# Order of the first heads of a fused attention and two-MLP kernel: six edits to its hand-written start

## The reference

```python
scores = q @ k.T / 8; scores = where(causal, -1e9, scores); scores -= scores.max(-1)
a = exp(scores); a /= a.sum(-1) + 1e-9
local = a @ v
phi = where(q > 0, q, exp(q) - 1) + 1
mem_out = (phi @ M_prev) / (phi @ z_prev + 1e-6)
x = g * mem_out + (1 - g) * local              # g = sigmoid(beta), per head
h = relu(x @ w_in); x = (s * h * h + b) @ w_out            # 2304 x 512, width 2048
h = x @ v_in; solu = h * softmax(h)                        # width 1024
out = layernorm(solu) * g_ln @ v_out
```

## Time and profile before

| | |
|---|---|
| median of three executions | 870.0 us |
| the profiled execution's own time | 870.0 us |
| its span, first to last instruction | 868.3 us |
| busy: TensorE, VectorE, ScalarE, GpSimd | 99%, 57%, 37%, 30% |
| granted TensorE clock, mean | 1.000 |
| TensorE waiting for VectorE's maxima (L948), whole span | 2.9 us in 7 waits |

### The profile page before, as it was taken

One profiled execution on the slowest core, in us unless ns is written; L12 is line 12 of the kernel. 1 busy time (PEld: TensorE's weight loads), 2 busy tenths in 40 slices (PEclk: granted clock), 3 DMA queues, 4 the chain that ended last, 5 costly groups with the idle time before them and its releaser, 6 DMA issues.

```text
span 868.3 us, 13401 instructions
## 1 busy us (share of the span) xinstructions
PE 855.3 (99%) x4966; PEld 755.7 (87%) x4966; DVE 492.5 (57%) x1036; ACT 317.6 (37%) x572; POOL 257.3 (30%) x371
## 2 busy tenths in 40 slices
PE   8999999999999999999999999999999999999998
PEld 7899999999888888888888889999998888888886
DVE  7766666666548865433443344344757655656664
ACT  6656566565432223222322222232243323232322
POOL 5656656565569992000000000000600000000000
PEclk9999999999999999999999999999999999999999
DMA  8665757564403322000000000000210000000000
GB/s 148 149 139 124 162 126 157 131 151 97 118 25 103 112 89 62 1 1 0 1 1 1 0 1 1 1 1 1 89 57 13 12 25 25 24 24 24 13 24 36
DMA packets 86359, 49.27 MB, mean 57 GB/s; under 512 B 65056, under 2 KB 73248, under 8 KB 86304
## 3 DMA queue, kind: packets, MB, share of 16 engines
q1 hardware_dynamic: 83760, 47.94, 22.8%
q10 hardware_dynamic: 2544, 0.59, 0.4%
HBM read 27.28 MB, written 4.72 MB: 37 GB/s over the span
## 4 chain that ended last, share of the span: by engine, by line
PE 89%; DVE 7%; issue 2%; ACT 1%; POOL 0%; POOLq 0%; ACTq 0%
PE ps_h L1265 8%; PE ps_h L1267 8%; PE ps_h L1266 8%; PE ps_y L1280 7%; PE ps_y L1282 7%; PE ps_y L1281 7%; PE ps_v L631 7%; PE ps_hid L1541 4%; PE ps_r L1570 4%; PE ps_s L546 4%; PE ps_hid L1543 4%; PE ps_hid L1542 4%; PE ps_r L1572 4%; PE ps_r L1571 4%; DVE spent L948 3%
## 5 line engine op out<-in xcount | busy, mean ns | idle before, releaser
L1384 DVE TENSOR_TENSOR xT<-xT 128x512 f32<-128x512 f32 (+1 forms) x80 | 60.3, 754 | 133.7 <-ACT xT L1340 133.7
L1265 PE MATMUL ps_h<-x_hi,win 128*128 128x512 f32 (+1 forms) x320 | 117.7, 368 | 0.0
L1267 PE MATMUL ps_h<-x_hi,win 128*128 128x512 f32 (+1 forms) x320 | 117.5, 367 | 0.0
L1282 PE MATMUL ps_y<-g_hi,wout 128*128 128x512 f32 (+1 forms) x320 | 117.5, 367 | 0.0
L1281 PE MATMUL ps_y<-g_lo,wout 128*128 128x512 f32 (+1 forms) x320 | 117.5, 367 | 0.0
L1266 PE MATMUL ps_h<-x_lo,win 128*128 128x512 f32 (+1 forms) x320 | 117.5, 367 | 0.0
L1280 PE MATMUL ps_y<-g_hi,wout 128*128 128x512 f32 (+1 forms) x320 | 117.4, 367 | 0.0
L631 PE MATMUL ps_v<-v_raw,pT 128*128 128x65 f32 (+1 forms) x960 | 107.6, 254 | 1.2 <-DVE t_loc L1046 1.2
L631 PEld LDWEIGHTS ps_v<-v_raw,pT 128*128 128x128 f32 (+1 forms) x960 | 101.3, 173 | 6.9 <-issue 4.7
L948 DVE CUSTOM_DVE_ANT_0 spent<-ps_s,mask 128x576 f32<-128x576 f32 (+4 forms) x160 | 81.6, 539 | 42.4 <-PE ps_s L546 41.6
L767 ACT ACTIVATE pT<-ps_x 128x512 f32<-128x512 f32 (+3 forms) x128 | 64.1, 501 | 94.5 <-PE ps_x L613 93.6
(11 more groups left out here) (164 smaller groups left out, 1685.7 us busy)
## 6 DMA issues: line engine op xcount, KB each, us to landing
stacked<-cut SPq DMA_DIRECT2D x56, 288.0 KB, 5.2
out<-res SPq DMA_DIRECT2D x18, 256.0 KB, 2.0
v_raw<-in_v SPq DMA_DIRECT2D x32, 128.0 KB, 3.2
stage<-in_moe_w_in SPq DMA_DIRECT2D x16, 256.0 KB, 2.7
stage<-in_moe_w_out SPq DMA_DIRECT2D x16, 256.0 KB, 2.6
k_raw<-in_k SPq DMA_DIRECT2D x28, 128.0 KB, 2.5
q_raw<-in_q SPq DMA_DIRECT2D x28, 128.0 KB, 3.6
stage<-in_moe_w_in SPq DMA_DIRECT2D x4, 512.0 KB, 3.8
```

The lines of the kernel that those rows point to most:

```text
L1265: pe.matmul(out, hi, x_hi[:, k, 0:n], start=(k == 0), stop=False)
L1267: ins = pe.matmul(out, lo, x_hi[:, k, 0:n], start=False, stop=(k == KT - 1))
L1282: ins = pe.matmul(out, wout[:, f, LO, w], g_hi[:, r, 0:n], start=False, stop=(f == FT - 1))
L1384: dve.tensor_tensor(r, r, r, ALU.mult).then_inc(square_done, 1)
```

## The change

Six edits, all in the written-out start.

1. GpSimd: `mask_weights(0, 1)` goes ahead of `spread_maxima(1)`, which now waits for 4 masked tiles, and `cut_queries(2)` ahead of `mask_weights(0, 3)`.
2. TensorE: `keep_warm` does twice as many matmuls where its output has fewer than 128 partitions, that is in its third call.
3. TensorE: `cross(0, 3)` goes ahead of `first_rows(2)`.
4. TensorE: `cross(3, 2)` goes behind `turn_queries(4)` and `third_rows(5)`.
5. VectorE: both `low_keys` of pair 1 go behind `first_rows(2)`.
6. VectorE: `second_rows(5)` goes ahead of `cut_keys(4)`.

```diff
--- before.py
+++ after.py
@@ -429,11 +429,11 @@
 
         mask_weights(0, 0)
         round_queries(2)
-        pool.wait_ge(q_hi_done, 1)
+        mask_weights(0, 1)
+        pool.wait_ge(tri_done, 4)
         spread_maxima(1)
-        mask_weights(0, 1)
+        cut_queries(2)
         mask_weights(0, 3)
-        cut_queries(2)
         features(0)
 
         mask_weights(1, 0)
@@ -481,7 +481,7 @@
                 pe.matmul(ps_s[:, 0:P], ident[:, :], ident[:, :], start=True, stop=True)
 
         def keep_warm(into):
-            for _ in range(WARM_BETWEEN):
+            for _ in range(WARM_BETWEEN * (2 if into.shape[0] < P else 1)):
                 pe.matmul(into, ident[:, 0:into.shape[0]], ident[:, :], start=True, stop=True)
 
         def turn_keys(p):
@@ -696,8 +696,8 @@
         turn_queries(2)
         third_rows(1)
         cross(0, 2)
+        cross(0, 3)
         first_rows(2)
-        cross(0, 3)
         turn_keys(2)
 
         cross(1, 0)
@@ -737,9 +737,9 @@
         second_rows(5)
         cross(3, 1)
         weigh_values(2, (2,))
-        cross(3, 2)
         turn_queries(4)
         third_rows(5)
+        cross(3, 2)
         weigh_values(2, (3,))
         cross(3, 3)
         memory(2)
@@ -1078,11 +1078,11 @@
         first_rows(1)
         low_queries(1, 1)
         second_rows(1)
+        third_rows(1)
+        first_rows(2)
+
         low_keys(1, 0)
-        third_rows(1)
         low_keys(1, 1)
-        first_rows(2)
-
         second_rows(2)
         cut_keys(2)
         third_rows(2)
@@ -1100,8 +1100,8 @@
         scale_local(0)
 
         first_rows(5)
+        second_rows(5)
         cut_keys(4)
-        second_rows(5)
         third_rows(5)
         scale_memory(2)
```

## The result

Six executions of the changed kernel took 874.13 to 878.68 us, median 875.35; six of the kernel before 869.97 to 870.48, median 870.25. The ratio is 1.0062, 95% interval 1.0046 to 1.0079. The forecast was 872.8, range 871.2 to 874.0: the direction held, the time lies outside. The spread is news too: 4.5 us, for 0.5 before. The profiled execution, a seventh, took 878.92 us, its span is 877.2. The fastest, 874.13 us, was the only one of the seven at full clock; its span is 871.2, so 2.9 us lie outside it, where the kernel before had 1.7.

A forecast was written before the change was run, and what follows sets the result against it. TensorE was taken to bound the loops, with only the first 48 us a chain of hand-overs. 1.49 us at the start plus 1.30 at pair 4 gave 2.79 on 870.0: forecast 872.8 us, range 871.2 to 874.0.

The forecast's parts named there:

- The replay of the hand-overs: First 48 us: same durations in the new order, hand-over latencies from neighbouring rows; lateness moves everything behind, sum 2.79 us.
- The doubled dummies: Third keep_warm, ahead of cross(0,0): five more matmuls make it 1.13 us later, bounds 0.76 and 1.13.
- the unnamed 0.37 us before 17.89: Gap on TensorE ahead of cross(0,0), not the old dummies' time; at most this could swallow new dummies.
- The low_keys: VectorE behind first_rows(2): 1.52 us for the pair, next maximum at 26.15 for 24.66, 1.49 us late; 0.34 without dummies.
- GpSimd's order: Last mask of head 0 late, weigh_values(0) stalls 0.83 us; costed at nothing, since TensorE has slack there.
- its cover is VectorE's lateness: The mask stall costs nothing because second_rows(3) waits for VectorE anyway; without that, up to 0.8 us.
- The second place: Pair 4, 44 to 48 us: cut_keys(4) late, turn_queries(4) at 47.18 for 46.23; costs 1.30 us, bounds 1.1 and 1.5.
- the first place: The start through heads 0 to 2, up to second_rows(3): all engines 1.49 us late, dummies included.
- the third rival: "The clock falls": new TensorE pauses bring half pace, 4 us of work lose 2; 874.8 us or more, chance 0.08.
- a pause of 0.96 us: Longest earlier TensorE pause counted, at 21.49, followed by full pace; set against new pauses of 0.5 to 1.4 us.
- Only one of the two places pays: Dummies hidden at the start, or VectorE far enough ahead at 44 us: 871.6 us, chance 0.14.
- not slower: Maxima first shortens VectorE's chain, shown by the 24.66 maximum starting before 24.7: 869.6 to 870.4 us, chance 0.08.

The follow-up runs named there:

- e13: The changed kernel run once more, beside three other kernels on one chip: median 876.73 us, ratio 1.0073, clock falls in 4 of 6.
- e4: The changed kernel with five dummy matmuls in each of two pauses, ahead of weigh_values(0) and turn_queries(4): median 873.25 us, no fall in 7.
- e14: The changed kernel with five dummies ahead of weigh_values(0) only, measured again on another chip: median 873.24 us, no fall in 6.
- e2: The kernel before with GpSimd's new order, cross(0,3) ahead of first_rows(2), low_keys behind it, single dummies: median 872.25 us, falls in 7 of 11.
- e5: The kernel before with only cross(3,2) moved behind turn_queries(4) and third_rows(5): median 870.62 us, ratio 0.9999, no fall in 11.
- e6: The kernel before with only second_rows(5) moved ahead of cut_keys(4) on VectorE: median 871.61 us, ratio 1.0010, no fall in 11.
- e1: The kernel before with only the third keep_warm doubled: median 871.16 us, ratio 1.0006, no fall in 11.
- e9: The changed kernel with five dummies ahead of weigh_values(0) only: median 873.10 us, ratio 1.0030, no fall in 6.
- e3: The kernel before with only cross(3,2) behind third_rows(5) and second_rows(5) ahead of cut_keys(4): median 873.4 us, ratio 1.0031, falls in 7 of 12.
- e16: The kernel before with only the cross(3,2) and second_rows(5) moves, measured again on another chip: median 873.87 us, ratio 1.0043, falls in 4 of 5.
- e11: The kernel before without its third keep_warm, the five dummies ahead of cross(0,0): median 871.89 us, ratio 1.0016, falls in 6 of 10.
- e12: The kernel before with pair 1's low_keys and gate operations in VectorE's waits, plus four TensorE moves of ready work into waits: median 869.52 us, ratio 0.9987.

## Why the prediction was wrong, step by step

**The replay of the hand-overs held in its places, and its sum partly by luck.** Sum 2.79; with the clock up the span grew by 2.8 (e13), and the medians of e4 and e14 lie 2.7 to 2.8 over the kernel before. But the start cost only 2.4, and 0.4 came in the first MLP, where the replay had nothing. By places:
- The doubled dummies: cross(0,0) 0.8 late, not 1.13. It was at the lower bound of 0.76: the unnamed 0.37 us before 17.89 did swallow dummies, and my reason for the upper end was wrong.
- The low_keys: VectorE's maximum 1.02 late, not 1.49. Most of the difference comes in with the dummies: first_rows(2) is at 22.14 where I had 22.42, the copy at 22.91 where I had 23.27; the low_keys behind it take their 1.52 us. Without the dummies I had 0.34; e2's executions with the clock up are 0.35 late in the middle.
- GpSimd's order: no cost of its own shows in time, as forecast, though no experiment has this edit alone. But the wait for the last mask (0.68 us) is the pause that went with the first fall, so "its cover is VectorE's lateness" was true for the hand-overs and false for the clock.
- The second place: turn_queries(4) 0.95 later than second_rows(3) was, and memory(2) 1.32; forecast 0.95 and 1.30. e5 and e6 divide it nearly as their texts said: 0.35 and 0.95, measured 0.1 and 1.05 in the medians.
- The last 0.4 us of the 2.8 come at 628 us. Up to there TensorE is 2.4 late in e13; then the first MLP's L1280 waits for VectorE, and the lateness is 2.8 from there on. VectorE is held up by one operation of 2.44 us, which takes 0.48 four microseconds later, while GpSimd is at a long one of its own:

```profile
626.73 2.58 POOL L1249 TENSOR_TENSOR win<-stage,win 128x1024 fp32r<-128x1024 f32 x1
627.09 2.44 DVE L1386 TENSOR_SCALAR xT<-xT,sb_in 128x384 f32<-128x384 f32 x1
...
630.74 0.44 PE L1280 MATMUL ps_y<-g_hi,wout 128*128 128x384 f32 x1 [0.17 <-DVE g_lo L1391]
```

In the kernel before GpSimd came to this operation 0.5 us later on that scale, having waited 0.69 us for a transfer, and there the long one on VectorE is L1391, and no matmul waited for it:

```profile
623.60 1.09 POOL L1246 TENSOR_SCALAR win<-stage 128x1024 fp32r<-128x1024 f32 x1 [0.69 <-DMA stage<-in_moe_w_in]
...
625.50 2.10 DVE L1391 TENSOR_TENSOR g_lo<-xT,g_hi 128x384 fp32r<-128x384 f32 x1 [0.59 <-ACT g_hi L1346]
```

e1, e9 and e14 have this 0.4 too, e3 and e16 don't. So what a late start costs can change far behind it, at a place that no edit touches. The replay passed lateness on unchanged, and here that was not so. Its sum came out at 2.8 since it had the first place 0.47 too dear.

**The step that failed is the third rival.** I gave "the clock falls" 0.08 and kept it out of the range, on the ground that a pause of 0.96 us was followed by full pace. It happened in 10 of 13 executions, and it accounts for 2.3 of the 2.55 us by which the median lies over the forecast (875.35, for 873.0 at full clock in e13). The row that I used was good evidence only for a pause of that length at that place. Its own cover, the dummies just ahead of it, I had priced as work and not as protection; e11 shows that the kernel before stands near this edge, since five dummies fewer make it fall in 6 of 10.

The rival's price, 2 us for one stretch and 874.8 or more, was about right for an execution at 0.998, which costs 2.2 us of span (873.4 to 871.2), and too low for the rest. In the execution of 877.2 us a stretch at 0.50 lasts some 7 us, not 4: second_rows(3) is 2.6 us behind that of e13 (35.23 and 32.19, less 0.42 for a later start), and the second place adds 2.9. That there could be two such stretches in one execution I had not seen.

The rule of the Trainium skill that I weighed ("TensorE: Matmul & The Clock Gate", "Part 1: The HAM clock gate") has the array at half rate after idleness. The changed kernel's trace agrees in this: waits of 0.38, 0.92 and 0.68 us, then 0.50; and with both pauses filled (e4) none of 7 fell. It was right to name it and wrong to give a trace without falls so much weight against it.

"Only one of the two places pays" and "not slower" are out: the maximum of 24.66 came at 25.68, and both pauses stand in both traces of the changed kernel.

## What to carry to other kernels

Where TensorE is the bound, price a new wait twice: by the hand-over that comes late, and by a stretch at half clock, here 1.3 to 3.5 us behind pauses of 0.7 to 1.2 us, in some executions and not in others. One profile cannot rule it out; look at the mean granted clock of every execution, and at the spread, and expect each later pause to move with the first fall. Follow the lateness to the end of the span: it can grow at a place that no edit touched. An order is improved by putting ready work into waits that exist (e12), and where a wait must stay, dummies in it cost little: second_rows(3) is at 32.37 in e4 and 32.19 in e13, and e4's median of 873.25 us is 0.1 to 0.2 above e13's two executions at full clock.

## What was not expected of the hardware

- One program with spans of 871.1 to 871.4 us at full clock, 873.4 and 873.5 at a mean of 0.998, and 875.6 to 877.2 at 0.992 to 0.994. In the execution traced at 877.2 the clock fell behind both pauses.
- The same pause of 1.2 us had falls or none according to its place: 11 of 17, none of 17 and 3 of 5 executions at three places 1.2 and 2.4 us apart. What in the chip decides it was not measured.
- The first 20 passes of dummies are busy for 4.09 us in e3's trace and 4.64 in e16's, the same kernel; the third dummies start 0.67 us apart (16.34 and 17.01), and the spans are 869.6 and 870.4. Between these two executions without a fall, the start makes most of the difference.
- Behind a stretch at half clock an idle wait was gone (second_rows(3) at 35.23 without one, for 0.57 us in e13), so a table of waits alone makes such an execution look better than its faster sister.
- VectorE's L1386 took 2.44 us beside a long operation of GpSimd and 0.48 without one; its L1391 took 2.10 beside one and 0.56 without. That the one slows the other was not tested by an experiment.
